# A fused attention, dense and expert kernel on one core: in the dense stage a pair's keys and queries are derived two slots sooner, ScalarE copies the states' products, and the token load is issued ahead of a clearing store

## The reference

```python
# attention: 4 batches, 8 heads, 768 steps, head size 48
for t in range(S):
    cur = np.einsum('bhd,bhe->bhde', u[None] * kt, vt)
    y[:, :, t] = np.einsum('bhd,bhde->bhe', rt, state + cur)
    state = wt[:, :, :, None] * state + np.einsum('bhd,bhe->bhde', kt, vt)
# dense: 3072 tokens x 384, hidden size 1024
h = (x @ w1) * (x @ w2) @ w3
x = h @ w_out
# experts: 8 experts, each token goes to its best two
noisy = x @ w_gate + log1p(exp(x @ w_noise)) * noise
# for each of the two chosen experts: relu(x @ w1[e]) @ w2[e], weighted and added
```

## Time and profile before

| | us |
|---|---|
| median of 3 runs (998.4, 1004.12, 1005.51) | 1004.12 |
| the profiled execution's own time | 999.43 |
| its span, first to last instruction | 997.7 |
| PE busy | 955.2 (96%) |
| DVE busy | 689.9 (69%) |
| ACT busy | 523.7 (52%) |
| mean granted TensorE clock | 0.990 |

### The profile page before, as it was taken

One profiled execution on the slowest core, in us unless ns is written; L12 is line 12 of the kernel. 1 busy time (PEld: TensorE's weight loads), 2 busy tenths in 40 slices (PEclk: granted clock), 3 DMA queues, 4 the chain that ended last, 5 costly groups with the idle time before them and its releaser, 6 DMA issues.

```text
span 997.7 us, 18088 instructions
## 1 busy us (share of the span) xinstructions
PE 955.2 (96%) x6825; PEld 902.0 (90%) x6825; DVE 689.9 (69%) x1161; ACT 523.7 (52%) x970; POOL 222.0 (22%) x209
## 2 busy tenths in 40 slices
PE   4999999999999999999999999999999999999995
PEld 3655999989998999999999999999999999999995
DVE  7889777879696978263778585765857658576570
ACT  2545444355453545234545575665756657566560
POOL 0000000110202020203344323333332432323311
PEclk8999999999999999999999999999999999999998
DMA  8986433352425220306348797877978779787751
GB/s 255 285 262 204 128 112 107 107 171 85 132 83 173 69 70 29 102 1 229 111 167 265 198 296 213 243 257 209 302 208 245 257 211 299 208 246 254 215 154 16
DMA packets 87307, 179.02 MB, mean 179 GB/s; under 512 B 18914, under 2 KB 44260, under 8 KB 87220
## 3 DMA queue, kind: packets, MB, share of 16 engines
q1 hardware_dynamic: 73844, 157.18, 49.5%
q0 software_dynamic: 12976, 20.66, 9.9%
q10 hardware_dynamic: 400, 0.02, 0.0%
HBM read 152.22 MB, written 26.97 MB: 180 GB/s over the span
## 4 chain that ended last, share of the span: by engine, by line
PE 80%; DVE 12%; issue 3%; ACT 2%; DMA 1%; SPq 0%; POOL 0%; DVEq 0%; ACTq 0%; POOLq 0%
PE bank L1209 20%; PE pp L1225 20%; PE bank L780 10%; PE bank L797 6%; PE fx L780 4%; PE yu L1268 3%; PE fx L797 3%; DVE kdiv L258 2%; PE pp L186 2%; PE tr L1190 2%; PE yu L1250 1%; PE fx L1250 1%; DVE work L865 1%; PE yu L230 1%; PE yu L207 1%
## 5 line engine op out<-in xcount | busy, mean ns | idle before, releaser
L1118 POOL DMA_INDIRECT result<-x2s,who x55 | 92.9, 1689 | 286.8 <-ACT x2s L1342 273.9
L1329 DVE SCALAR_TENSOR_TENSOR abl<-bank,abh 128x512 fp32r<-128x512 f32 x96 | 66.2, 690 | 109.9 <-ACT abh L1324 109.9
L969 POOL DMA_INDIRECT slot_entry<-entry,slot_i x48 | 50.3, 1048 | 352.9 <-DVE token_f L958 340.7
L1209 PE MATMUL bank<-xh,set_up_h 128*128 128x256 f32 x384 | 109.2, 284 | 0.0
L1209 PE MATMUL bank<-xh,set_up_l 128*128 128x256 f32 x384 | 108.6, 283 | 0.0
L1209 PE MATMUL bank<-xl,set_up_h 128*128 128x256 f32 x384 | 108.6, 283 | 0.0
L1324 ACT ACTIVATE abh<-bank 128x512 fp32r<-128x512 f32 x96 | 57.5, 599 | 81.3 <-PE bank L1209 81.2
L780 PE MATMUL bank<-xh,w12h 128*128 128x384 f32 x264 | 89.7, 340 | 1.4 <-DVE xl L477 0.9
L780 PE MATMUL bank<-xh,w12l 128*128 128x384 f32 x264 | 88.4, 335 | 0.0
L780 PE MATMUL bank<-xl,w12h 128*128 128x384 f32 x264 | 88.2, 334 | 0.0
L1225 PE MATMUL pp<-set_down_h,abh 128*128 128x384 f32 x256 | 87.7, 342 | 0.0
(11 more groups left out here) (260 smaller groups left out, 2650.5 us busy)
## 6 DMA issues: line engine op xcount, KB each, us to landing
up_raw<-in_moe_w SPq DMA_DIRECT2D x93, 512.0 KB, 4.6
down_raw<-in_moe_w SPq DMA_DIRECT2D x124, 384.0 KB, 4.8
vs<-in_v_rows SPq DMA_DIRECT2D x16, 384.0 KB, 3.4
wt<-in_w SPq DMA_DIRECT2D x32, 144.0 KB, 2.8
kt<-in_k SPq DMA_DIRECT2D x32, 144.0 KB, 2.8
rt<-in_r SPq DMA_DIRECT2D x32, 144.0 KB, 3.0
kn<-in_k_rows SPq DMA_DIRECT2D x16, 288.0 KB, 3.3
rn<-in_r_rows SPq DMA_DIRECT2D x16, 288.0 KB, 4.8
```

The lines of the kernel that those rows point to most:

```text
L969: nc.gpsimd.indirect_dma_start(slot_entry, bass.IndirectOffsetOnAxis(slot_i[:, s, n:n + 1], 0), entry[:, s, n, :], None).then_inc(scattere ...
L1118: nc.gpsimd.indirect_dma_start(out, bass.IndirectOffsetOnAxis(who[v % 4][:, s, 0:1], 0), yo[v % 2][:, s, 0:DM], None, bounds_check=N - 1, ...
L1209: last = nc.tensor.matmul(bank[m % 2][:, f * T2:(f + 1) * T2], wp[:, kk, c:c + P], xp[:, kk, :], start=(n == 0), stop=(n == 3 * KD - 1))
L1329: nc.vector.scalar_tensor_tensor(hl[:, 2 * m:2 * m + 2, :].rearrange("p a t -> p (a t)"), bank[m % 2][:, :], 0.0, hh[:, 2 * m:2 * m + 2, : ...
```

## The change

Four edits, which come down to this. In the dense stage the reciprocals' second and third thirds, the keys and the queries (`derive` 2 to 5) go from slots 5, 6, 7, 8 to slots 4, 5, 6, 7. The second and third step of the diagonal (`diag` 1 and 2) go from slots 4 and 5 to 5 and 6. The weight stage keeps its slots. The copy of the states' products moves from DVE to ACT, in both stages. The turn of the next batch's first group goes one down step later. On SP the token load of a batch's first group goes ahead of the clearing store and of that store's wait, the clearing goes behind the second output half and the load of values, and SP no longer waits for the token load to land.

```diff
         def dve_state(dve, b, q):
             g = HP * b + q
-            dve.wait_ge(yu_full, 3 * g + 1)
-            need(dve, state_ready, (NC - 1) * (g - 1))
-            nc.vector.tensor_copy(added[q % 2][:, :, :], yu[:, 0:(NC - 1) * D].rearrange("p (c x) -> p c x", c=NC - 1)
-                                  ).then_inc(yu_free, 1)
             dve.wait_ge(yu_free, g + 1)
...
+        def act_products(act, b, q):
+            g = HP * b + q
+            act.wait_ge(yu_full, 3 * g + 1)
+            nc.scalar.copy(added[q % 2][:, :, :], yu[:, 0:(NC - 1) * D].rearrange("p (c x) -> p c x", c=NC - 1)
+                           ).then_inc(yu_free, 1)
...
-        def pair_slots(q, first=False):
+        def pair_slots(q, first=False, weights=False):
...
-                     [("out", q, 0), ("out", q, 1)],
-                     [("derive", q + 1, 2)],
-                     [("derive", q + 1, 3)], [("derive", q + 1, 4)], [("derive", q + 1, 5)], []]
-            for part, at in enumerate((3, 4, 5) if first else (0, 4, 5)):
+                     [("out", q, 0), ("out", q, 1)], [], [], [], [], []]
+            for part, at in enumerate((5, 6, 7, 8) if weights else (4, 5, 6, 7)):
+                slots[at].append(("derive", q + 1, part + 2))
+            for part, at in enumerate(((3, 4, 5) if first else (0, 4, 5)) if weights else (0, 5, 6)):
                 slots[at].append(("diag", q + 1, part))
             for part, at in enumerate((6, 7, 8, 9)):
                 slots[at].append(("spread", q + 1, part))
...
-            if step == "scale":
+            if step == "state":
+                act_products(act, b, q)
+            elif step == "scale":
...
-            TURN_AT = 4
+            TURN_AT = 5
...
                             sp_attention(sp, b + 1, step, q, n)
-                            if n == 0:
+                            if (q, n) == (HP - 1, 0):
+                                sp_group_load(sp, b + 1, 0)
+                            if n == 1:
                                 sp_clear(sp, HP * b + q)
                                 sp.wait_ge(zeros_stored, 16 * (HP * b + q + 1))
-                            if (q, n) == (HP - 1, 0):
-                                sp_group_load(sp, b + 1, 0)
-                                sp.wait_ge(xr_loaded[0], 16 * (b + 2))
```

More of the change, by code:

```diff
@@ L501, in program @@
             order = threaded(front, first_slots())
-            order += threaded(build, [slot for q in range(HP) for slot in pair_slots(q, q == 0)] + [[]] * TAIL)
+            order += threaded(build, [slot for q in range(HP) for slot in pair_slots(q, q == 0, True)] + [[]] * TAIL)
             sums = (fx, bank[1])
```

## The result

| | before | changed |
|---|---|---|
| median of 20 runs each | 1002.21 us (998.4 to 1006.87) | 994.83 us (993.73 to 1000.23) |
| ratio changed / before | | 0.9935 [0.9921, 0.995] |
| the profiled execution's own time, its span | 999.43, 997.7 | 997.37, 995.6 |

By the ratio the change saves 6.5 us of 1002 (5.0 to 7.9); the two medians differ by 7.4. The forecast was 996.5, from 5.4 less. So the stages are compared by their lengths, and the totals by the timed runs.

What follows compares the result with a forecast made beforehand. The prediction took PE as the bound, with only 7.8 us idle in the dense stage to win. Its terms, 0.7 (mask), 3.9 (batch ends) and 0.8 (copy), sum to 5.4 us less, giving 996.5 us, range 990 to 1003.

Steps and rivals of the forecast that it cites:

- The bound: Whole kernel: PE, busy 96% of the span, bounds it; only its 7.8 us idle in the dense stage can be won.
- the clock takes no part: Dense stage: the granted clock is 1.00 there, so it was given no term.
- The second third of the reciprocals: Dense stage, DVE before 165.97: 1.67 us of work fits an idle stretch of 2.43 us, so it costs nothing.
- The diagonal and the new wait: Dense stage, up 11: the sum 2.4 us later holds ACT's copy of up 8; new PE wait of about 0.65 us.
- The mask's waits: Dense stage, second half of scores: five waits of 0.79 go, 0.65 replaces each; 0.14 a site, 0.7 us in all.
- The batch ends: Ends of batches 0 and 1: keys and queries come sooner, so the first half of scores stops waiting; 3.9 us less.
- The copy: Weight stage: products copied by ACT in 0.37 us move three chains up by 0.28 each; 0.8 us less.
- The sum: Whole kernel: 0.7 + 3.9 + 0.8 = 5.4 us less, taken from a mean of 1001.9: 996.5 us.
- ACT is not blocked: Rival, dense stage: no new wait, the whole 7.8 comes back with 0.8 from the weight stage; 993.3 us, chance 0.15.
- The gain is eaten: Rival: wait at up 11 is 1.3 us and one batch end falls to another late item; 1002 us, chance 0.19.
- The tokens share the DMA engines: Rival, batch ends: tokens land late beside stores and loads, 6.9 us slower; 1008.8 us, chance 0.08.

Runs made afterwards that it cites:

- sum_sooner: Changed kernel with the diagonal's second and third step back in slots 4 and 5 of the dense stage; 990.44 us, ratio 0.9888 to before, dense stage 304.53 us.
- before_b: Second profiled execution of the kernel before, nothing changed; dense stage 317.96 us, against 312.98 in the first.
- ends_only: Kernel before with only the token load ahead of the clearing and the turn one down step later; 995.91 us, ratio 0.9939, dense stage 308.94 us.
- before_c: Third profiled execution of the kernel before, nothing changed; dense stage 313.26 us.
- changed_b: Second profiled execution of the changed kernel, nothing altered; dense stage 308.44 us, against 308.43 in the first.

## Why the prediction was right

**The bound.** That only PE's 7.8 us of idle time in the dense stage could be won is a little low even for an execution that kept its clock: sum_sooner won 8.5 there, since a wait costs more than the idle time that it shows. The sentence "the clock takes no part" failed. It was read from one profile with 1.00 throughout; before_b has 0.50 behind both batch ends. There, waits of 1.9 and 2.4 us had 1.6 and 2.9 us of lost clock behind them. No term of the sum stood for that. It would have the size of 6.5 against 5.4, but 5.4 lies inside the measured 5.0 to 7.9, so this is not shown.

**The second third of the reciprocals.** Costed at nothing, and up 5's product still had 1.72 us of idle time in front of it. Right.

**The diagonal and the new wait.** Right in place, number (five), releaser and reason. Its size was right too, for what was worked out: up 11 was forecast to start about 0.65 late and started 0.63 late. But the idle time shown for that is 0.47, and the cost 0.74. The mask's waits, counted as 0.79, cost 0.86: up 13 starts 4.21 us before up 14 where they stand, and 3.35 where they don't. So both prices were too low, the new one by about a tenth, and the difference between them, 0.14 forecast, came out at 0.12. Five sites give 0.6; batch 0's first group, where no new wait was counted, takes 0.15 of it back. The slots' own part is 0.5 us (ends_only less the changed kernel) instead of 0.7. The swap was the weakest part of the change: it traded one wait for another, and sum_sooner shows that neither was needed.

**The batch ends.** Forecast 3.9, measured 4.0 (ends_only). The tokens were forecast to land within 5 us; the moved loads took 4.2 to 4.4 in the three kernels that show them. What I didn't see is that two sets of edits do the same work, that SP's order is not needed for it, and that the later turn, which the forecast gives no term of its own, has a part in both.

**The copy.** Forecast 0.37 us on ACT, measured 0.36. Forecast three chains of 0.28: of the first 0.3 is shown, the second can't be told from its scatter, and what the third gains is given back before up 0, which waits for `xl` then. So 0.3 to 0.65 instead of 0.8. The row of the Trainium skill that was weighed there (page "ScalarE: Activation LUTs", section "Rules for kernel authors") names relu, max, min, add and mul and gives its figure for bf16. This copy, f32 out of PSUM, is neither, and took 0.36 us on ACT beside 0.39 on DVE.

**The sum.** Dense stage 4.6 forecast and 4.5 measured, weight stage 0.8 and 0.3 to 0.65: about 5. The timed difference is 6.5 (5.0 to 7.9). So the terms fit the profiles better than the total, and the total is right by its interval; what fills the gap is not settled beyond the clock's possible part. The 996.5 itself also leaned on the mean of four executions, 1001.9, which happened to be close to the median of the twenty, 1002.21.

**The rivals.** *ACT is not blocked* is refuted by the row at 177.09. *The gain is eaten* too: the new wait is smaller than the old, and both ends came free. *The tokens share the DMA engines* would have needed landings of over 7 us; of the nine moved loads seen, with 912 KB issued behind each on the same queue, the slowest took 4.4. In the changed kernel ACT began on the tokens of the first batch end 5.4 us after their issue, and PE didn't wait.

## What to carry to other kernels

A step that another engine's strict queue waits for should be moved with that queue in hand: ask what stands behind its first consumer, since a ready copy there waits too. Test a bundle's parts alone: here the later turn with the sooner load gave nearly all, the slots repeated most of it, and the sum's later place took back most of what the sooner keys and queries gave. Price a wait by the starts of the work around it, and not by the idle time shown. And when a kernel's executions scatter, look at the granted clock of each before looking for a cause in the code; behind a wait of 2.4 us on TensorE another 2.9 were lost here in one execution of three.

## What the runs showed of the hardware

- A wait of TensorE costs more than the idle time shown: 0.47 shown was 0.74 between the starts of the up steps, 0.79 was 0.86.
- The same wait of 2.4 us (2.36 to 2.48) was followed by a clock of 0.50 for nearly 7 us in one execution and by none in two others. In the final stage two executions, before_c and changed_b, lost the clock for some 3 us behind a wait of 1.85 and 1.84 us; before_b had the same wait, 1.85, and kept it. This is changed_b, in the windows from the wait on:

```profile
518.00:520.00 2.00, 0.82 (x7) 0.82 (x7) 1.32 (x2) 2.00 (x4) 1.58 (x2) 1.00 0.94 162
520.00:522.00 2.00, 2.00 (x14) 2.00 (x13) 2.00 (x3) 0.77 (x1) 1.44 (x1) 0.62 1.00 258
522.00:524.00 2.00, 2.00 (x10) 2.00 (x10) 1.28 (x3) 1.60 (x3) 0.00 (x0) 0.52 0.82 293
```

- That wait, for DVE's `abl` (L1333 in the changed kernel), was 0 in the first profile of either kernel and 1.6 to 2.7 us in the four later ones. Why was not tried. It stays open, with the landings of `w3T` (0 to 4.3 us of waits in the weight stage).
